# Gate logits with the token blocks as the loaded operand instead of the gate's weights

## Chip, cores and metric

One NeuronCore of a Trainium2 chip runs the whole program. The metric is the device time of one launch in microseconds (us); lower is better.

## What is computed

Three stages in a row, all in fp32 at the interface:

```python
# 1: attention with a memory term: q, k, v of [2, 8, 576, 64]; x becomes [1152, 512]
# 2: a dense layer pair
h = x @ w_in                              # [1152, 2048]
x = softplus(h) @ w_out                   # [1152, 512]
# 3: a mixture of 8 experts, weighted by a balanced matrix
logits = x @ w_gate                       # [1152, 512] @ [512, 8]
P = np.exp(logits - logits.max())
for _ in range(8):
    P /= P.sum(1, keepdims=True) + 1e-09
    P /= P.sum(0, keepdims=True) + 1e-09
    P *= N / E
for e in range(E):
    out += P[:, e:e + 1] * (np.maximum(x @ w1[e], 0.0) @ w2[e])
```

The case is about `logits = x @ w_gate`, the product of 1152 tokens by 8 experts, and about what stands around it in time.

## The kernel before, in words

**Stages.** TensorE works through the attention of 8 pairs of heads, then stage 2 in 2 groups of hidden features by 3 chunks of 384 tokens (N1 = 384), then stage 3. The output of stage 2 is `y1`, laid out with the 512 features on partitions (4 tiles `kt` of 128) and the 1152 tokens along the free axis; it lies in the buffer that is later `acc`, so the trace calls it acc.

**Stage 3.** Every expert is two halves, every half four units u = 0 to 3. The products of x and w1 (`hidden2`) are Strassen-like: seven products "P1" to "P7" of sums of blocks. Units 0 and 1 take tokens 0 to 511 (operands xah, xal, 256 columns wide), units 2 and 3 take tokens 512 to 1151 (operands xbh, xbl, 320 columns wide). Each fp32 product is made of three fp32r products of high and low parts (`products`, line 1525). The result goes to the second product (`output2`, pieces "T0" to "T4", loaded operand zh or zl, 512 columns of w2c moving).

**The order is written out by hand.** TensorE runs, for each unit, the pieces P1, P6, P5, T0, P2, P7, T1, P3, T2, P4, T3, T4, where the P pieces are already those of the next unit and the T pieces those of this one. Each engine has its own list in the same spirit, and they meet at semaphores. Of those that matter here: P2 of a unit waits for `s1_done` (ScalarE has copied P1 out of its bank, `take_s1`), P7 for `u2_done` (VectorE's `sum_u2`, which needs that copy), P6 of the next unit for `h21_done`.

**The gate.** After the last piece of unit 0's hidden product (P3 and P4) TensorE waits for `ld_g` (the gate's weights have landed) and for `y_drained` (VectorE has added the last chunk into y1) and makes the logits expert by token (lines 1757 to 1764): 3 chunks of 384 tokens by 4 feature tiles, 12 matmuls in fp32, the loaded operand being 8 columns of w_gate and the moving one 384 tokens. Chunk 0 goes to the bank `bank_sk` (half of ps_g), chunks 1 and 2 to two banks of ps_y. ScalarE copies the three chunks to `logit_t` in the buffer h_work (`copy_logits`, between the splits `tokens_b` of the operands xbh), each copy signalled in `g_copied`. In the first unit, after piece P5, TensorE waits for all three copies, transposes nine blocks of 8 by 128 back to token by expert in bank_sk (line 1792), and signals `g_tok`. VectorE then takes the maximum (line 1432), further small steps on TensorE (after P7 and P3) and VectorE spread it over the partitions, and ScalarE takes the exponential (line 1043) that the eight balancing rounds start from. `output2` of unit 0 waits for `g_copied` too, since its banks held logits.

**The sums beside it.** While TensorE makes the logits, GpSimd makes four sums of token blocks in order (`token_sums`, lines 663 to 668, tile xbs), ScalarE copies seven operands to xbh (`tokens_b` 0, 1, 2, 3, 4, 6, 5; the last needs the fourth sum) and only then runs `take_s1` of unit 1; VectorE makes the low parts xbl.

```python
            tokens_b(0)
            copy_logits(0)
            tokens_b(1)
            tokens_b(2)
            copy_logits(1)
            tokens_b(3)
            copy_logits(2)
            tokens_b(4)
            tokens_b(6)
            tokens_b(5)
```

Of the kernel before, what the change touches and what calls it, by code (L numbers as in the profile page):

```python
# [13 lines left out]
P = 128  # L14
# [57 lines left out]
def build(nc, q, k, v, M_prev, z_prev, beta, moe_w_in, moe_w_out, moe2_w_gate, moe2_w1, moe2_w2, out):  # L72
    B, H, S, D = q.shape
    DM = H * D
    KT = DM // P
    T = B * S
    E = moe2_w1.shape[0]
# [9 lines left out]
    G1 = moe_w_in.shape[1] // FS  # L87
    C1 = 3
    N1 = T // C1
    NTT = T // P  # L90
# [24 lines left out]
    with ExitStack() as top:  # L115
        def sem(name):
            return top.enter_context(nc.semaphore(name))
# [5 lines left out]
        def at_(name, offset, shape, dt=F32):  # L123

            size = SIZE[dt] * math.prod(shape[1:])
            end = offset + (size + 31) // 32 * 32
            assert end <= LIMIT, (name, end)
            return nc.alloc_sbuf_tensor_at(name, shape, dt, offset=offset), end

        ident, o = at_("ident", BASE, [P, P])  # L130
# [41 lines left out]
        for g in range(G):  # L172
            t_, o = at_(f"pth{g}", o, [P, 2, GKEYS[g], GCOLS[g][1] - GCOLS[g][0]], F32R)
            pth.append(t_)
        for g in range(G):
            t_, o = at_(f"ptl{g}", o, [P, 2, GKEYS[g], GCOLS[g][1] - GCOLS[g][0]], F32R)
# [17 lines left out]
        h_work, o = at_("h_work", X1, [P, 4, N1])  # L194
# [7 lines left out]
        y1 = acc[:, :, :].rearrange("p a b -> p (a b)").rearrange("p (k t) -> p k t", k=KT)  # L202
# [40 lines left out]
        wg, o = at_("wg", o, [P, KT, E])  # L243
# [9 lines left out]
        assert o <= W20 + 5 * DM * 4  # L253
        zh[1], o = at_("zh1", o, [P, 2, 2 * NB], F32R)
        zl[1], o = at_("zl1", o, [P, 2, 2 * NB], F32R)
        logit_t = h_work[0:E, :, :].rearrange("p a b -> p (a b)")

        with ExitStack() as at:
            ps_s = at.enter_context(nc.psum_tensor("ps_s", [P, 4, 512], F32))
# [3 lines left out]
        with ExitStack() as ml:  # L263
            ps_h = ml.enter_context(nc.psum_tensor("ps_h", [P, 2, 512], F32))
            ps_y = ml.enter_context(nc.psum_tensor("ps_y", [P, KT, 512], F32))
            ps_g = ml.enter_context(nc.psum_tensor("ps_g", [P, 2, 512], F32))
        bank_a, bank_b, bank_c = ps_h[:, 0, :], ps_g[:, 0, :], ps_h[:, 1, :]
        bank_sk = ps_g[:, 1, :]
# [16 lines left out]
        def z_bank(u, k):  # L285
            if u < 2:
                return ps_y[:, k, :]
            return bank_sk if k == 0 else ps_y[:, k - 1, :]
# [52 lines left out]

        y_ready = sem("y_ready")
        y_drained = sem("y_drained")
        g_ready = sem("g_ready")
        g_copied = sem("g_copied")
        g_tok = sem("g_tok")
        g_max = sem("g_max")
        g_row = sem("g_row")
# [385 lines left out]
        def _(act):  # L734
# [12 lines left out]
            copy = lambda o, i, **kw: act.activation(o, i, ACT.Copy, **kw)  # L747
# [231 lines left out]
                    act.wait_ge(z_drained, ZT + i + 1)  # L979
                    act.activation(acc[:, i, :], acc[:, i, :], ACT.Copy, scale=weight[:, i, 0:1]).then_inc(scaled, 1)  # L980

            def copy_logits(c):
                act.wait_ge(g_ready, c + 1)
                copy(logit_t[0:E, c * N1:(c + 1) * N1], (bank_sk if c == 0 else ps_y[:, c - 1, :])[0:E, 0:N1])\
                    .then_inc(g_copied, 1)

            def tokens_b(x):
                tokens_hi(x, 2 * NA, NB, xbh, xbs, xb_sum, xb_hi)

# [9 lines left out]
            relu_hi(0, 0, "21")  # L999
            act.wait_ge(y_drained, KT * G1 * C1 + KT)  # L1000
            tokens_b(0)
            copy_logits(0)
            tokens_b(1)
            tokens_b(2)
            copy_logits(1)
            tokens_b(3)
            copy_logits(2)
            tokens_b(4)
            tokens_b(6)
            tokens_b(5)  # L1010
# [469 lines left out]
        def _(pe):  # L1480
# [41 lines left out]
            def products(dst, a, b, start, stop):  # L1522

                for i, (x, y) in enumerate(((0, 0), (0, 1), (1, 0))):
                    last = pe.matmul(dst, a[x], b[y], start=start and i == 0, stop=stop and i == 2)  # L1525
                return last
# [177 lines left out]
            def output2(s, u, k, start):  # L1704

                U, i = 4 * s + u, u % 2
                if k == 0:
                    pe.wait_ge(e_lo, 4 * U + 4)
                    if u < 2:
                        pe.wait_ge(c2_lo, 2 * s + i + 1)  # L1710
                if i == 0:
                    if u == 0:
                        if start:
                            pe.wait_ge(g_copied, min(k + 2, C1))
                        else:
                            pe.wait_ge(z_drained, ZT * s + k - 3)
                    elif k == 0:
                        if start:
                            pe.wait_ge(g_exp, 1)
                        else:  # L1720
                            pe.wait_ge(z_drained, ZT * s - 4)
                    else:
                        pe.wait_ge(z_drained, ZT * s + k)
                cols = slice(k * P, (k + 1) * P)
                for f in range(2):
                    last = products(z_bank(u, k), (zh[u % 2][:, f, cols], zl[u % 2][:, f, cols]),
                                    (w2c_h[i][:, f, :], w2c_l[i][:, f, :]), i == 0 and f == 0, i == 1 and f == 1)
                if k == (TA if u < 2 else TB) - 1:
                    last.then_inc(unit_done, 1)
                elif i == 1:  # L1730
                    last.then_inc(z_ready, 1)
# [23 lines left out]
            hidden2(0, 0, ("P3", "P4"))  # L1755

            pe.wait_ge(ld_g, 16)
            pe.wait_ge(y_drained, KT * G1 * C1 + KT)
            for c in range(C1):
                bank = bank_sk if c == 0 else ps_y[:, c - 1, :]  # L1760
                for kt in range(KT):
                    last = pe.matmul(bank[0:E, 0:N1], wg[:, kt, :], y1[:, kt, c * N1:(c + 1) * N1],  # L1762
                                     start=kt == 0, stop=kt == KT - 1)
                last.then_inc(g_ready, 1)

            def column_sums(it, U):

                if SK_AT[it][1] == "P7":
                    pe.wait_ge(h11_done, U + 2)
                else:  # L1770
                    pe.wait_ge(t12_done, U + 2)
                pe.wait_ge(sk, 8 * it + 4)
                pe.matmul(sums_at(it), ones[:, :], weight[:, :, :].rearrange("p t e -> p (t e)"),
                          start=True, stop=True).then_inc(sk_sum, 1)


            def expert(e, first, last):
                for half in range(2):
                    s, final = 2 * e + half, last and half == 1
                    start = first and half == 0  # L1780
                    for u in range(4):
                        for piece in ("P1", "P6", "P5", "T0", "P2", "P7", "T1", "P3", "T2", "P4", "T3", "T4"):
                            if piece[0] == "T":
                                k = int(piece[1])
                                if k < (TA if u < 2 else TB):
                                    output2(s, u, k, start)
                            elif not (final and u == 3):
                                hidden2(s + (u == 3), (u + 1) % 4, (piece,))
                            if start and u == 0 and piece == "P5":
                                pe.wait_ge(g_copied, C1)  # L1790
                                for i in range(NTT):
                                    t_ = pe.transpose(bank_sk[:, i * E:(i + 1) * E], logit_t[0:E, i * P:(i + 1) * P],
                                                      ident[0:E, 0:E])
                                t_.then_inc(g_tok, 1)
                            if start and u == 0 and piece == "P7":
                                pe.wait_ge(g_max, 1)
                                pe.transpose(bank_sk[0:1, 2 * P:3 * P], sk_max[:, 0:1], ident[:, :]).then_inc(g_row, 1)
                            if start and u == 0 and piece == "P3":
                                pe.wait_ge(g_max, 2)
                                pe.matmul(bank_sk[:, 3 * P:3 * P + 1], ones[0:1, :], sk_max[0:1, 1:2],  # L1800
                                          start=True, stop=True).then_inc(g_all, 1)
                            if first and (4 * s + u, piece) in SK_AT:
                                column_sums(SK_AT.index((4 * s + u, piece)), 4 * s + u)

            expert(0, True, False)
            with pe.Fori(1, E - 1) as e:
                expert(e, False, False)
            expert(E - 1, False, True)


# [21 lines left out]
```

## Time and profile before

| what | value |
|---|---|
| median of 3 runs | 1111.4 us (1110.64 to 1111.64) |
| the profiled execution's own time | 1110.8 us |
| its span, first to last instruction | 1109.0 us |
| TensorE matmuls busy | 1097.5 us (99% of the span), 6698 of them |
| TensorE weight loads busy | 999.2 us (90%) |
| VectorE, ScalarE, GpSimd busy | 704.7, 488.1, 435.2 us |
| mean granted TensorE clock | 1.000 |

PE is TensorE's matmul side and PEld its side that loads the stationary operand; the two overlap. In a row of the trace "ps_y<-acc,wg 128*8 128x384" the output comes first, then the moving operand, then the loaded one; 128*8 is the size of the loaded operand (rows by columns) and 128x384 that of the moving one. An fp32 matmul (as against fp32r) shows as two loads and two matmuls. The ends of matmuls are modelled, so starts of neighbouring rows say more than their durations.

### The profile page before, as it was taken

Reading aid. Unit: us, or ns where it says so; the run is one execution under the profiler, and the core shown is the slowest. Engines: PE = TensorE matmul, PEld = TensorE weight load, DVE = VectorE, ACT = ScalarE, POOL = GpSimd, SP = SyncE. Lnnn points to the kernel's source line nnn. Section 1 sums busy time; section 2 is a strip of 40 time slices with the busy share of each in tenths; the row PEclk is TensorE's granted clock in tenths of the full one; section 3 lists DMA queues with packets and bytes.
Section 4 is the critical chain, followed back from the end, with each engine's and each line's share of the span. In section 5 each row is a group of like instructions: output and inputs, shape, how many; then the busy total and the mean of one; then the engine's idle time right before and its main releaser. Section 6 shows DMA issues by size and latency. Waiting matters only on the chain.

```text
span 1109.0 us, 20425 instructions
## 1 busy us (share of the span) xinstructions
PE 1097.5 (99%) x6698; PEld 999.2 (90%) x6698; DVE 704.7 (64%) x1327; ACT 488.1 (44%) x1069; POOL 435.2 (39%) x486
## 2 busy tenths in 40 slices
PE   7999999999999999999999999999999999999998
PEld 5888999999997989899899898999989898898987
DVE  7999743453278787675756656566665666756564
ACT  6888765664565333433333333333233332333331
POOL 7899700001044334352442524335343442524421
PEclk9999999999999999999999999999999999999999
DMA  5433202001001110111101011110111101111001
GB/s 122 107 96 94 69 29 76 1 27 51 0 20 39 38 58 20 58 58 39 49 27 57 35 41 56 38 57 19 57 57 38 57 19 57 57 38 40 19 10 76
DMA packets 66061, 52.78 MB, mean 48 GB/s; under 512 B 32608, under 2 KB 54112, under 8 KB 66016
## 3 DMA queue, kind: packets, MB, share of 16 engines
q1 hardware_dynamic: 65728, 52.20, 15.3%
q8 instruction: 25, 0.41, 0.2%
q14 instruction: 20, 0.16, 0.0%
q10 hardware_dynamic: 288, 0.01, 0.0%
HBM read 49.83 MB, written 2.36 MB: 47 GB/s over the span
## 4 chain that ended last, share of the span: by engine, by line
PE 95%; DVE 2%; issue 1%; POOL 1%; SPq 1%; DMA 0%; ACT 0%; POOLq 0%; DVEq 0%
PE ps_y L1525 40%; PE ps_h L1525 27%; PE ps_g L1525 17%; PE ps_o L1525 4%; PE ps_p L1567 2%; PE ps_s L1541 2%; PE ps_s L1525 1%; PE ps_y L1762 0%; POOL prob L625 0%; DVE zl L1282 0%; PE ps_t L1505 0%; DVE acc L1402 0%; PE ps_t L1517 0%; PE ps_g L1762 0%; PE ps_t L1510 0%
## 5 line engine op out<-in xcount | busy, mean ns | idle before, releaser
L936 ACT ACTIVATE zh<-h 128x256 fp32r<-128x256 f32 (+1 forms) x256 | 112.2, 444 | 329.4 <-POOL h L698 134.1
L1525 PE MATMUL ps_y<-w2c_h,zh 128*128 128x512 f32 x512 | 202.7, 396 | 0.0
L1525 PE MATMUL ps_y<-w2c_l,zh 128*128 128x512 f32 x512 | 201.8, 394 | 0.0
L1525 PE MATMUL ps_y<-w2c_h,zl 128*128 128x512 f32 x512 | 199.3, 389 | 0.0
L693 POOL TENSOR_TENSOR h<-u,p 128x256 f32<-128x256 f32 (+1 forms) x64 | 56.9, 890 | 362.0 <-DVE u L1259 362.0
L1282 DVE SCALAR_TENSOR_TENSOR zl<-h,zh 128x256 fp32r<-128x256 f32 (+1 forms) x256 | 173.0, 681 | 8.6 <-ACT zh L936 8.5
L1525 PEld LDWEIGHTS ps_y<-w2c_h,zl 128*128 128x128 f32 x512 | 96.2, 188 | 21.9
L1525 PEld LDWEIGHTS ps_y<-w2c_h,zh 128*128 128x128 f32 x512 | 96.6, 189 | 13.5
L1525 PEld LDWEIGHTS ps_y<-w2c_l,zh 128*128 128x128 f32 x512 | 96.6, 189 | 11.8
L1410 DVE SCALAR_TENSOR_TENSOR acc<-ps_y,weight,acc 128x512 f32<-128x512 f32 x112 | 82.0, 741 | 37.2 <-PE ps_y L1525 37.2
L698 POOL TENSOR_TENSOR h<-h,p 128x256 f32<-128x256 f32 (+1 forms) x64 | 60.9, 952 | 101.7 <-DVE h L1270 101.7
L1212 DVE SCALAR_TENSOR_TENSOR h_work<-ps_h,h_work 128x384 f32<-128x384 f32 x48 | 26.7, 557 | 94.4 <-ACT h_work L870 94.4
L1525 PE MATMUL ps_h<-xbh,w1c_l 128*128 128x320 f32 x256 | 79.1, 309 | 0.0
L1525 PE MATMUL ps_h<-xbl,w1c_h 128*128 128x320 f32 x256 | 79.0, 308 | 0.0
L1525 PE MATMUL ps_h<-xbh,w1c_h 128*128 128x320 f32 x256 | 78.6, 307 | 0.0
L686 POOL TENSOR_TENSOR w1c_l<-ws,w1c_h 128x1024 fp32r<-128x1024 f32 x32 | 77.0, 2407 | 0.0
L1525 PE MATMUL ps_h<-xah,w1c_l 128*128 128x256 f32 x256 | 72.4, 283 | 0.0
L1525 PE MATMUL ps_h<-xal,w1c_h 128*128 128x256 f32 x256 | 72.4, 283 | 0.0
L1525 PE MATMUL ps_h<-xah,w1c_h 128*128 128x256 f32 x256 | 72.1, 282 | 0.0
L677 POOL TENSOR_TENSOR ws<-rc 128x256 f32<-128x256 f32 x32 | 25.7, 802 | 117.5 <-DMA rc<-in_moe_w_dram 116.0
L1276 DVE TENSOR_TENSOR h<-ps_g,u 128x256 f32<-128x256 f32 (+1 forms) x64 | 29.3, 458 | 64.5 <-PE ps_g L1525 64.3
L747 ACT ACTIVATE s<-ps_h 128x256 f32<-128x256 f32 (+1 forms) x64 | 26.2, 410 | 96.9 <-PE ps_h L1525 96.8
(248 smaller groups left out, 3031.8 us busy)
## 6 DMA issues: line engine op xcount, KB each, us to landing
rc<-in_moe_w_dram SPq DMA_DIRECT2D x64, 512.0 KB, 3.6
out_dram<-acc SPq DMA_DIRECT2D x9, 256.0 KB, 2.0
q_nat<-in_q_dram SPq DMA_DIRECT2D x16, 128.0 KB, 2.5
k_nat<-in_k_dram SPq DMA_DIRECT2D x16, 128.0 KB, 2.7
v_nat<-in_v_dram SPq DMA_DIRECT2D x16, 128.0 KB, 2.4
raw<-in_moe_w_in_dram SPq DMA_DIRECT2D x8, 256.0 KB, 3.0
raw<-in_moe_w_out_dram SPq DMA_DIRECT2D x8, 256.0 KB, 3.2
raw<-in_moe_w_in_dram SPq DMA_DIRECT2D x1, 2048.0 KB, 8.7
```

The costliest lines, as they stand in the source:

```text
L677: pool.tensor_tensor(ws[:, 0, :, :], a21, a22, ALU.add).then_inc(c1_sum, 1)
L686: pool.tensor_tensor(w1c_l[i][:, 3:7, :, :], ws[:, :, :, :], w1c_h[i][:, 3:7, :, :].bitcast(F32), ALU.subtract).then_inc(c1_los, 1)
L693: pool.tensor_tensor(h22[:, 0:n], u3[:, 0:n], p5[:, 0:n], ALU.add).then_inc(h22_done, 1)
L698: pool.tensor_tensor(h12[:, 0:n], h12[:, 0:n], p5[:, 0:n], ALU.add).then_inc(h12_done, 1)
L747: copy = lambda o, i, **kw: act.activation(o, i, ACT.Copy, **kw)
L936: act.activation(z_place(u, quarter, 0), rows, ACT.Relu).then_inc(e_hi, 1)
L1212: dve.scalar_tensor_tensor(out=h_sp[:, slot % 2, :], in0=ps_h[:, slot % 2, 0:N1], scalar=0.0, in1=h_abs[:, slot % 2, :], op0=ALU.max, op1= ...
L1276: dve.tensor_tensor(h21[:, 0:n], bank_b[:, 0:n], u3[:, 0:n], ALU.add).then_inc(h21_done, 1)
L1282: dve.scalar_tensor_tensor(out=z_place(u, quarter, 1), in0=rows[:, 0:n], scalar=0.0, in1=z_place(u, quarter, 0).bitcast(F32), op0=ALU.max, ...
L1410: dve.scalar_tensor_tensor(out=here, in0=y, scalar=weight[:, i, bass.ds(e, 1)], in1=here, op0=ALU.mult, op1=ALU.add).then_inc(z_drained, 1)
L1525: last = pe.matmul(dst, a[x], b[y], start=start and i == 0, stop=stop and i == 2)
L1541: pe.matmul(ps_s[:, bank + h, 0:w], x[r, half, t * P:(t + 1) * P], y[r, half, 0:w], start=i == 0, stop=False)
```

## The change

The logits are made token by expert at once: for each of the nine blocks of 128 tokens, the block of y1 (128 by 128) is the loaded operand and the 8 columns of w_gate move, 4 feature tiles each, so 36 matmuls. All go to bank_sk, where the transposes used to put their result. The wait for the last chunk of y1 is moved to the first block that reads it (block 6), `g_tok` is signalled by the last matmul, and the copies, the transposes, the buffer view and the two semaphores go.

```diff
-        logit_t = h_work[0:E, :, :].rearrange("p a b -> p (a b)")
...
-            def copy_logits(c):
-                act.wait_ge(g_ready, c + 1)
-                copy(logit_t[0:E, c * N1:(c + 1) * N1], (bank_sk if c == 0 else ps_y[:, c - 1, :])[0:E, 0:N1])\
-                    .then_inc(g_copied, 1)
...
             tokens_b(0)
-            copy_logits(0)
             tokens_b(1)
             tokens_b(2)
-            copy_logits(1)
             tokens_b(3)
-            copy_logits(2)
             tokens_b(4)
...
                     if u == 0:
-                        if start:
-                            pe.wait_ge(g_copied, min(k + 2, C1))
-                        else:
+                        if not start:
                             pe.wait_ge(z_drained, ZT * s + k - 3)
...
             pe.wait_ge(ld_g, 16)
-            pe.wait_ge(y_drained, KT * G1 * C1 + KT)
-            for c in range(C1):
-                bank = bank_sk if c == 0 else ps_y[:, c - 1, :]
+            for i in range(NTT):
+                if i * P == T - N1:
+                    pe.wait_ge(y_drained, KT * G1 * C1 + KT)
                 for kt in range(KT):
-                    last = pe.matmul(bank[0:E, 0:N1], wg[:, kt, :], y1[:, kt, c * N1:(c + 1) * N1],
+                    last = pe.matmul(bank_sk[:, i * E:(i + 1) * E], y1[:, kt, i * P:(i + 1) * P], wg[:, kt, :],
                                      start=kt == 0, stop=kt == KT - 1)
-                last.then_inc(g_ready, 1)
+            last.then_inc(g_tok, 1)
...
-                            if start and u == 0 and piece == "P5":
-                                pe.wait_ge(g_copied, C1)
-                                for i in range(NTT):
-                                    t_ = pe.transpose(bank_sk[:, i * E:(i + 1) * E], logit_t[0:E, i * P:(i + 1) * P],
-                                                      ident[0:E, 0:E])
-                                t_.then_inc(g_tok, 1)
```

## Rows read from the trace of the kernel before

**Rows 1.** The page: TensorE's share, and the chain that ended last by engine.
```profile
PE 1097.5 (99%) x6698; PEld 999.2 (90%) x6698; DVE 704.7 (64%) x1327; ACT 488.1 (44%) x1069; POOL 435.2 (39%) x486
PE 95%; DVE 2%; issue 1%; POOL 1%; SPq 1%; DMA 0%; ACT 0%; POOLq 0%; DVEq 0%
```

**Rows 2.** Groups by line, TensorE: logits (L1762), transposes (L1792); busy us, mean ns.
```profile
L1762 PE MATMUL ps_y<-acc,wg 128*8 128x384 f32 x16 | 5.3, 486 | 0.0
...
L1792 PE MATMUL ps_g<-ident,h_work 8*128 8x8 f32 x9 | 0.7, 204 | 0.0
```

**Rows 3.** Timeline, TensorE, both ends of the logits: start us, us, engine, line.
```profile
342.55 0.28 PE L1525 MATMUL ps_g<-xah,w1c_l 128*128 128x256 f32 x1
342.76 0.10 PEld L1762 LDWEIGHTS ps_g<-acc,wg 128*8 128x8 f32 x2
...
349.86 0.09 PEld L1762 LDWEIGHTS ps_y<-acc,wg 128*8 128x8 f32 x1 [0.23 <-issue]
350.60 0.19 PEld L1525 LDWEIGHTS ps_h<-xah,w1c_h 128*128 128x128 f32 x1 [0.65 <-issue]
```

**Rows 4.** Timeline, TensorE: P5's last matmul, the transposes, T0, P2's first.
```profile
352.62 0.28 PE L1525 MATMUL ps_h<-xal,w1c_h 128*128 128x256 f32 x1
352.74 0.28 PE L1525 MATMUL ps_h<-xah,w1c_l 128*128 128x256 f32 x1
352.95 0.63 PEld L1792 LDWEIGHTS ps_g<-ident,h_work 8*128 8x128 f32 x9
...
353.60 0.19 PEld L1525 LDWEIGHTS ps_y<-w2c_h,zh 128*128 128x128 f32 x1
...
354.86 0.19 PEld L1525 LDWEIGHTS ps_h<-xah,w1c_h 128*128 128x128 f32 x1
355.09 0.28 PE L1525 MATMUL ps_h<-xah,w1c_h 128*128 128x256 f32 x1
```

**Rows 5.** Timeline, TensorE: a small fp32 matmul with a full 128x128 load.
```profile
372.88 0.33 PEld L1773 LDWEIGHTS ps_h<-weight,ones 128*128 128x128 f32 x2
...
373.13 0.19 PEld L1525 LDWEIGHTS ps_y<-w2c_h,zh 128*128 128x128 f32 x1
...
373.24 0.19 PEld L1525 LDWEIGHTS ps_y<-w2c_l,zh 128*128 128x128 f32 x1
```

**Rows 6.** Timeline, ScalarE: a logit copy, the last xbh, take_s1.
```profile
350.71 0.48 ACT L747 ACTIVATE h_work<-ps_y 8x384 f32<-8x384 f32 x1 [1.47 <-PE ps_y L1762]
...
353.39 0.74 ACT L747 ACTIVATE xbh<-xbs 128x640 fp32r<-128x640 f32 x1 [0.95 <-POOL xbs L668]
354.03 0.37 ACT L747 ACTIVATE s<-ps_h 128x256 f32<-128x256 f32 x1
```

**Rows 7.** Timeline, GpSimd's last sum and VectorE's first steps behind it.
```profile
351.21 2.15 POOL L668 TENSOR_TENSOR xbs<-acc 128x640 f32<-128x640 f32 x1
...
354.43 0.42 DVE L1253 TENSOR_TENSOR u<-ps_g,s 128x256 f32<-128x256 f32 x1 [0.39 <-ACT s L747]
...
356.00 0.42 DVE L1264 TENSOR_TENSOR h<-ps_h,s 128x256 f32<-128x256 f32 x1 [0.28 <-PE ps_h L1525]
...
362.50 0.41 DVE L1276 TENSOR_TENSOR h<-ps_g,u 128x256 f32<-128x256 f32 x1
```

**Rows 8.** Windows: us, busy (x) of PE, PEld, DVE, ACT, POOL, PEclk, DMA, GB/s.
```profile
7.00:8.00 1.00, 0.88 (x6) 0.64 (x6) 0.69 (x1) 0.26 (x2) 0.00 (x0) 1.00 0.84 190
8.00:9.00 1.00, 0.00 (x0) 0.00 (x0) 0.60 (x1) 1.00 (x3) 0.00 (x0) 1.00 0.27 58
...
1105.00:1106.00 1.00, 0.73 (x4) 0.27 (x2) 0.39 (x2) 0.00 (x0) 0.00 (x0) 1.00 0.36 139
...
1108.00:1109.00 1.00, 0.00 (x0) 0.00 (x0) 0.00 (x0) 0.00 (x0) 0.00 (x0) 0.55 0.07 25
...
342.60:350.60 8.00, 8.00 (x27) 2.11 (x26) 7.32 (x6) 4.19 (x8) 7.78 (x5) 1.00 0.01 2
```

**Rows 9.** Timeline, TensorE, the first ten matmuls of the program (512 columns each).
```profile
1.54 4.41 PE L1487 MATMUL ps_s<-idle 128*128 128x512 f32 x10 [1.54 <-POOL idle L545]
```

More of the change, by code:

```diff
@@ L343, in build @@
         y_drained = sem("y_drained")
-        g_ready = sem("g_ready")
-        g_copied = sem("g_copied")
         g_tok = sem("g_tok")
```

## The prediction

> **What bounds the kernel now.** I read the page first: TensorE's matmul side is busy 99% of the span and the chain that ended last is 95% TensorE [rows 1]. So time is won only where TensorE's own row of work gets shorter, and lost wherever it waits. The engines beside it count only through waits. Next I read the groups by line, which put a price on what is replaced: the 12 fp32 logit matmuls are 24 records, of which the 16 in ps_y are busy 5.3 us, and 0.7 us for the nine transposes [rows 2]. Then the timeline around both places, because modelled ends overlap and only the starts tell what the path pays. The windows come last, for TensorE's clock.
>
> **Old cost on TensorE's path.** The logits' first load starts at 342.76 and the first load of the next piece at 350.60: 7.84 us [rows 3], or 0.32 us for each of 24 records. That is 384 columns taken twice over at 2.4 GHz, so the streaming of the tokens is the bound and the 8-column loads are idle most of the time ("issue" 0.23 us before each). The entry before it costs little: the last matmul of P4 starts at 342.55, and at the 0.12 us spacing of such 256-column matmuls (352.62 to 352.74 in [rows 4]) the logits could have come at 342.67, so two waits cost 0.09 us. The transposes: P5's last matmul starts at 352.74, where T0's first load would lie if nothing came between (loads start with the matmul ahead of them, 373.13 and 373.24 in [rows 5] being the spacing when nothing hides them). It lies at 353.60 [rows 4]. So transposes and their waits take 0.86 us, of which 0.63 is the nine loads.
>
> **New cost.** 36 fp32 matmuls show as 72 loads of 128 columns and 72 matmuls of 8. The moving side is next to nothing: by the old block's own rate, 0.32 us x 8/384 = 0.007 us. The load becomes the bound. The trace before has no stretch of such pairs, but the nearest rows are close: the column sums of the balancing, fp32, 128x128 loaded, 72 columns moving. Two loads take 0.33 us together at 0.19 each, so the second starts at 373.02; the next load starts at 373.13 and the one after at 373.24 [rows 5]. A full fp32 load follows a small matmul every 0.11 us. 72 x 0.11 = 7.92 us; with the rounding of the rows, 0.106 to 0.112 each, 7.6 to 8.1 us. I take 7.9, against 7.84 before: **the block itself gains nothing**, at best 0.2 and at worst costs 0.3 us. The wait for y_drained moved into it costs what it cost in front of it.
>
> The Trainium skill, in "TensorE: Matmul & The Clock Gate", section "Back-to-back issue gap", gives a measured pace of about 81 ns for load and matmul pairs at 128 columns. By that pace the block would be 72 x 0.081 = 5.8 us, an estimate from the page. The 0.11 us of the fp32 load here disagrees with it, and the measured row decides.
>
> **What the removed parts give.** The transposes go: 0.86 us off TensorE's row. The three copies go from ScalarE, about 0.4 to 0.5 us each [rows 6]; at 350.71 the copy was the last of them, behind an idle 1.47 us. This gives no time by itself, since ScalarE's next deadline is set elsewhere: its last xbh copy waited 0.95 us for GpSimd's fourth sum, which ends at 351.21 + 2.15 = 353.36 [rows 6, 7]. Neither GpSimd's sums nor VectorE's work there wait for logits. g_tok comes 3 us earlier, but VectorE takes the maximum in its list behind sum_u2, which runs at 354.43 when ScalarE's copy is there [rows 7]; nothing follows. No DMA is added, removed or moved.
>
> **What is late next.** P2 of unit 1 needs ScalarE's copy of P1, which starts at 354.03, behind the xbh copy, and ends at 354.40 [rows 6]; with some 0.05 us of signalling, P2's load can start at about 354.45. Before, that load started at 354.86 [rows 4], so there was 0.4 us of slack. With 0.86 us gone and the block 0.08 longer, TensorE would come to it at 354.08 and now waits about 0.4 us; its load, hidden before, then stands open, and the matmul follows at 354.45 + 0.11 = 354.56 instead of 355.09 [rows 4]. **So 0.5 us is what arrives, and it is a cap**: the GpSimd chain does not move with TensorE, however fast the logits get. It also means that a block up to 0.4 us longer than I take costs nothing. Behind it VectorE was waiting for TensorE (0.28 us at 356.00), so it moves up by about that; result_21 at 362.50 + 0.41 [rows 7] would end near 362.65, in time for P6 of unit 2, which came at 363.6 less 0.5. From there on VectorE has waits for TensorE again and the lead is kept to the end.
>
> **The sum.** Block +0.08, transposes -0.86, new wait for ScalarE +0.25 net: -0.53 us. Against the profiled execution's 1110.8 us (span 1109.0 and 1.8 around it) that is 1110.3. That execution lies 0.6 us under the median of the runs, 1111.4; so the median to expect is **1110.9 us**. About 0.2%, 2.2 us, is what a measurement of this kernel can tell from no change, so this is "the same". Its own range is 1110.2 to 1111.7: the bounds of the block, plus the scatter of the runs shown (1.0 us).
>
> **Rivals.**
>
> *A: the clock falls (slower).* In the new block TensorE loads all the time but streams about 0.007 us in 0.11, for 8 us on end. The rows before have no such stretch: the logits ran at a granted clock of 1.00 with the matmul side streaming throughout [rows 8]. They do show that idleness brings the clock to its 1.2 GHz level: the last matmuls end at about 1105.7, and 1108 to 1109 has a mean of 0.55 [rows 8], so the clock fell at about 1108.1, 2.4 us after. And they show what recovery takes: the first ten matmuls take 4.41 us, (4.41 - 0.62 for the last)/9 = 0.42 us each for 512 columns, which is the 1.2 GHz level (1.54 us in, [rows 9]), so some 4 us of dense work come before full speed. Price: if it falls 2.4 us into the block, the remaining 5.5 us cost as much again, and 4 us of dense work afterwards cost 2 more; if it falls at the block's very end, only those 2. With the 0.86 us gained: +1.2 to +6.7, middle +4, so 1115.4 us (1112.6 to 1118.1). It decides on whether loading counts as work for the clock. For: by streaming alone the block is nearly idle. Against: loads and matmuls are under way in every moment of it; and in 7 to 9 us the clock stayed at 1.00 with few 128-column transposes and then a whole idle microsecond [rows 8]. Two bounds and no row between them: 0.43.
>
> The Trainium skill, same page, "Part 4: PE-mode transpose", says that transposes do not count as busy for the clock as matmuls do. The 1.00 over 7 to 9 us does not bear that out, since only transposes stood there; but by such a rule a stretch of loads with hardly any stream would count for little too, and give rival A's time.
>
> *B: the load is quicker than I take (faster).* The nine loads of the transposes take 0.63 us, 0.07 each [rows 4]. At that pace the block is 72 x 0.07 = 5.0 us and TensorE is 0.86 + 2.8 = 3.7 us early. But then P2 waits for the same copy at 354.40, and the gain is still 0.5 us. To get over 2.2 us, GpSimd's chain would have to speed up by 1.7 as well, for which nothing speaks. 0.03.
>
> *C: load and matmul do not overlap.* Then each pair costs up to 0.11 + 0.1 us for the matmul to get through, the block is 15 us and the time 1118. Against: in [rows 4] nine pairs with 8 moving columns run at 0.07 us although each matmul lasts 204 ns [rows 2], so they do overlap. 0.02.
>
> *D: the change doesn't do what it says.* That the block still shows 24 records, or copies remain; the diff leaves no room. Under 0.01.
>
> **How the numbers follow.** Forecast (same) 0.52, A 0.43, C 0.02, B 0.03. A's lowest part (a fall late in the block) would count as same, but the forecast has a tail above as well; I leave same at 0.53, slower 0.44, faster 0.03. The predicted time is the forecast's. The range needs both cases: from 1110.2 to 1116.8 it leaves out the lowest twentieth of the forecast, the top fifth of A and C.
>
> **What the profile after would show.** 72 loads and 72 matmuls on the new line, from about 342.7 to 350.6, starts 0.11 us apart; no L747 copies of h_work; T0's load straight after P5; a wait of P2 for ScalarE of 0.3 to 0.5 us near 354; the span near 1108.5. If A is right: granted clock under 1.00 in the window from 342.6 to 360, loads 0.2 us apart from some point on, 256-column matmuls 0.24 us apart after. I am wrong if the block is not load-bound, or if the stall at P2 is absent while the 0.86 us show up whole.

## The result: slower by half a per cent, and the profile after

| | before | changed |
|---|---|---|
| median, 6 runs each | 1111.2 us (1110.64 to 1111.64) | 1116.29 us (1115.13 to 1117.04) |
| ratio | | 1.0045, 95% interval 1.0032 to 1.0058 |
| span of the profiled execution | 1109.0 us | 1115.2 us |
| mean granted TensorE clock | 1.000 | 0.993 |

5.1 us were lost where 0.5 were forecast to be won. The profiled execution of the changed kernel is the slowest of its six (1117.04 us), so its span is 6.2 us longer than the one before, not 5.1. The page of the changed kernel, TensorE's part and the granted clock in 40 slices:

```profile
PE 1102.9 (99%) x6737; PEld 1010.8 (91%) x6737; DVE 704.3 (63%) x1327; ACT 487.0 (44%) x1066; POOL 435.1 (39%) x486
PEclk9999999999997999999999999999999999999999
PE 95%; DVE 2%; issue 1%; SPq 1%; POOL 1%; DMA 1%; ACT 0%; POOLq 0%; DVEq 0%
```

By shares and chain next to nothing has changed against [rows 1]: TensorE is still busy 99% of the span and still is 95% of the chain. The one line that differs is the granted clock, in its thirteenth slice. The windows around it, changed kernel (us, then busy of PE, PEld, DVE, ACT, POOL, then PEclk, DMA share, GB/s):

```profile
342.60:345.00 2.40, 2.40 (x24) 2.40 (x23) 1.56 (x5) 0.74 (x3) 1.61 (x2) 1.00 0.05 15
345.00:347.00 2.00, 2.00 (x16) 2.00 (x16) 2.00 (x2) 1.86 (x3) 2.00 (x2) 0.77 0.00 0
347.00:349.00 2.00, 2.00 (x11) 2.00 (x11) 2.00 (x2) 0.74 (x1) 1.92 (x2) 0.50 0.00 0
...
355.00:357.00 2.00, 2.00 (x11) 2.00 (x11) 0.00 (x0) 0.00 (x0) 0.00 (x0) 0.50 0.00 0
357.00:360.00 3.00, 3.00 (x17) 3.00 (x17) 0.81 (x3) 0.38 (x1) 0.00 (x0) 0.54 0.00 0
360.00:365.00 5.00, 5.00 (x33) 4.40 (x31) 2.93 (x7) 2.17 (x4) 0.79 (x1) 1.00 0.00 0
```

From the means the clock drops to its 1.2 GHz level at 346.1 (0.77 over 345 to 347) and is back at 2.4 GHz at 359.8 (0.54 over 357 to 360): 13.7 us at the low level. The counts of instructions say it too: 24 matmuls and 23 loads in the first 2.4 us, 11 of each in 2 us once the clock is low. Busy shares say nothing, all of them are full. TensorE's timeline of the same stretch:

```profile
343.29 0.28 PE L1514 MATMUL ps_g<-xah,w1c_l 128*128 128x256 f32 x1
343.29 12.94 PEld L1749 LDWEIGHTS ps_g<-wg,acc 128*128 128x128 f32 x72
...
356.11 0.33 PEld L1514 LDWEIGHTS ps_h<-xah,w1c_h 128*128 128x128 f32 x1
...
358.46 0.42 PE L1514 MATMUL ps_g<-xal,w1c_h 128*128 128x256 f32 x1
358.67 0.42 PE L1514 MATMUL ps_g<-xah,w1c_l 128*128 128x256 f32 x1
...
359.86 0.19 PEld L1514 LDWEIGHTS ps_y<-w2c_h,zh 128*128 128x128 f32 x1
...
361.13 0.19 PEld L1514 LDWEIGHTS ps_h<-xah,w1c_h 128*128 128x128 f32 x1
361.36 0.28 PE L1514 MATMUL ps_h<-xah,w1c_h 128*128 128x256 f32 x1
368.97 0.31 PE L1514 MATMUL ps_h<-xbh,w1c_h 128*128 128x320 f32 x1
```

The 72 loads take 12.8 us, from 343.29 to the next load at 356.11; in [rows 3] the block took 7.84. A narrower window of the weight loads shows the first part at full clock, 25 loads in 2.91 us or (2.91 - 0.19)/24 = 0.113 us each:

```profile
343.29 2.91 PEld L1749 LDWEIGHTS ps_g<-wg,acc 128*128 128x128 f32 x25
```

The other 47 take (356.11 - 343.29 - 25 x 0.113)/47 = 0.213 us each, 1.9 times as long. The 256-column matmuls behind are 0.21 us apart (358.46, 358.67) instead of 0.12, 1.8 times as long. So the loads slow down with the clock nearly as much as the matmuls do, and neither takes quite twice as long. Once the clock is back, T0 to P2 run as they should, and nothing idles ahead of P2 (its load at 361.13): TensorE is by then so late that ScalarE's copy has long been made.

For an account that leaves the scatter of the attention stage out (0.7 us in these two profiles, 342.55 against 343.29), I take one stretch in all kernels below: from the last matmul of P4 (before: 342.55 in [rows 3]; changed: 343.29) to the first 320-column matmul, unit 2's P1. Before it is at

```profile
362.73 0.30 PE L1525 MATMUL ps_h<-xbh,w1c_h 128*128 128x320 f32 x1
```

so the stretch is 20.18 us before and 368.97 - 343.29 = 25.68 us changed, 5.50 more. The rest of the program is as long as before (1109.0 - 362.73 = 746.3 and 1115.2 - 368.97 = 746.2).

### The profile page after: what moved, and what is told of

Same layout as the page of the kernel before. It is cut to its first block, busy times and chain, and to the rows that moved or that the text cites. A ratio compares the mean times of both kernels' runs of the same rounds, so it can differ in the third digit from the quotient of the medians.

```text
span 1115.2 us, 20499 instructions
## 1 busy us (share of the span) xinstructions
PE 1102.9 (99%) x6737; PEld 1010.8 (91%) x6737; DVE 704.3 (63%) x1327; ACT 487.0 (44%) x1066; POOL 435.1 (39%) x486
## 4 chain that ended last, share of the span: by engine, by line
PE 95%; DVE 2%; issue 1%; SPq 1%; POOL 1%; DMA 1%; ACT 0%; POOLq 0%; DVEq 0%
PE ps_y L1514 40%; PE ps_h L1514 27%; PE ps_g L1514 17%; PE ps_o L1514 4%; PE ps_p L1556 2%; PE ps_s L1530 2%; PE ps_g L1749 1%; DMA mem_nat<-in_M_prev_dram 1%; PE ps_s L1514 0%; DVE zl L1271 0%; PE ps_t L1494 0%; DVE acc L1391 0%; PE ps_t L1506 0%; PE ps_t L1499 0%; SPq L449 0%
```

## The experiments

Theory 1: the clock falls because next to nothing streams through TensorE while it loads. Theory 2: it is the kind or number of instructions (8 us of full fp32 loads), however many columns they stream. The forecast's own steps, a block of 7.9 us and a gain capped by a wait for ScalarE, wanted a test as well.

### Streaming more without doing more

The loaded operands, instructions and waits stay as in the change; the moving operand is repeated R times, its copies written side by side in the same bank and never read.

```diff
-                    last = pe.matmul(bank_sk[:, i * E:(i + 1) * E], y1[:, kt, i * P:(i + 1) * P], wg[:, kt, :],
+                    last = pe.matmul(bank_sk[:, 0:R * NTT * E].rearrange("p (r c) -> p r c", r=R)[:, :, i * E:(i + 1) * E],
+                                     y1[:, kt, i * P:(i + 1) * P], wg[:, kt, :].unsqueeze(1).to_broadcast([P, R, E]),
                                      start=kt == 0, stop=kt == KT - 1)
```

R = 7, 56 columns, expected:

> The changed kernel, but each logit matmul moves the gate's 8 columns seven times over (56 columns, seven copies side by side in the same bank; only the first is read). Loads, instructions, order and waits are those of the changed kernel. Theory 1 (the clock falls because almost nothing streams): streaming 56 columns takes 0.05 us (0.32 x 56/384) and stays hidden behind the 0.11 us load, the clock stays at 1.00, the block takes 7.9 us as forecast, first load of the block to first load of T0 is 10.0 us (before 10.84, changed 16.57), median 1110.4 to 1111.0. Theory 2 (the clock falls because of 8 us of back-to-back full fp32 loads, or of so many short instructions, whatever they stream): the clock falls as in the changed kernel, first load to T0 16 to 17 us, median about 1116.3. If theory 1 holds it also shows whether P2 of unit 1 waits for ScalarE's copy at all: forecast a matmul start 0.2 to 0.3 us later than the 0.23 us spacing of T0's matmuls would give.

Measured: 1110.85 us, before beside it 1110.78, ratio 0.9998 (0.9988 to 1.0008). One of its ten runs took 3178.32 us at a mean clock of 1.00; nothing on record says why, and the ratio leaves it out. Windows of its profile, 344 to 352 us, of which the two in the middle read 1.00 as well, and the timelines of TensorE and ScalarE:

```profile
344.00:346.00 2.00, 2.00 (x21) 2.00 (x19) 1.57 (x1) 2.00 (x5) 2.00 (x1) 1.00 0.00 0
...
350.00:352.00 2.00, 2.00 (x20) 2.00 (x20) 2.00 (x2) 0.65 (x2) 2.00 (x2) 1.00 0.00 0
```
```profile
343.00 0.28 PE L1514 MATMUL ps_g<-xah,w1c_l 128*128 128x256 f32 x1
343.12 8.14 PE L1749 MATMUL ps_g<-wg,acc 128*128 128x56 f32 x72
...
354.47 0.39 PE L1514 MATMUL ps_y<-w2c_h,zl 128*128 128x512 f32 x1
355.00 0.35 PE L1514 MATMUL ps_h<-xah,w1c_h 128*128 128x256 f32 x1
...
362.69 0.30 PE L1514 MATMUL ps_h<-xbh,w1c_h 128*128 128x320 f32 x1
```
```profile
343.00 8.13 PEld L1749 LDWEIGHTS ps_g<-wg,acc 128*128 128x128 f32 x72
351.05 0.19 PEld L1514 LDWEIGHTS ps_h<-xah,w1c_h 128*128 128x128 f32 x1
...
353.19 0.19 PEld L1514 LDWEIGHTS ps_y<-w2c_h,zh 128*128 128x128 f32 x1
...
354.24 0.19 PEld L1514 LDWEIGHTS ps_y<-w2c_h,zl 128*128 128x128 f32 x1
354.97 0.19 PEld L1514 LDWEIGHTS ps_h<-xah,w1c_h 128*128 128x128 f32 x1 [0.54 <-issue]
```
```profile
353.85 0.74 ACT L744 ACTIVATE xbh<-xbs 128x640 fp32r<-128x640 f32 x1 [1.38 <-POOL xbs L665]
354.49 0.37 ACT L744 ACTIVATE s<-ps_h 128x256 f32<-128x256 f32 x1
```

The same 72 loads and the same number of matmuls, more columns, and the clock stays at 1.00 over the block: theory 2 is out. It is not one execution's luck: the mean clock of the whole run was 0.998 to 1.000 in all ten runs here, and 0.992 to 0.995 in the six of the changed kernel. The block takes 8.05 us (343.00 to 351.05), 0.112 per load, and the stretch 362.69 - 343.00 = 19.69 us, 0.49 less than before; the forecast was 0.53. The median does not show it: a gain of this size is within the interval. The idle 0.54 us ahead of P2's load is the wait that was forecast, at about 0.4: ScalarE's copy s runs from 354.49 to 354.86, behind the xbh copy that waited for GpSimd, and the load follows at 354.97.

R = 3, 24 columns, expected:

> The same with three copies (24 columns moving, 0.02 us of streaming per 0.11 us load). Theory 1 expects something between the changed kernel (8 columns, fell) and the one with 56: most likely the clock still falls and the time is 1115 to 1117. Theory 2: falls as in the changed kernel, 1116.3. If it does not fall, 1110.4 to 1111.0, little streaming is enough.

Measured: a single run, 1115.47 us (before 1110.78). The clock falls, 5.6 us after the first load (343.36 to 348.9) instead of 2.8. With one profile of each, it is not shown that the columns make it later:

```profile
346.00:348.00 2.00, 2.00 (x21) 2.00 (x20) 2.00 (x2) 0.93 (x2) 2.00 (x2) 1.00 0.00 0
348.00:350.00 2.00, 2.00 (x16) 2.00 (x15) 2.00 (x2) 0.74 (x1) 1.90 (x2) 0.73 0.00 0
350.00:352.00 2.00, 2.00 (x11) 2.00 (x11) 2.00 (x2) 0.74 (x1) 1.95 (x1) 0.50 0.00 0
```

R = 5, 40 columns, together with the step of ScalarE's list that is told below, expected:

> As the 56-column version with ScalarE's step moved, but five copies of the gate's columns (40 moving). If the clock stays at 1.00 it is the same as with 56 columns, since the load of 0.11 us is the bound in both: first logit load to first 320-column matmul 19.3 us, median 0.3 to 0.85 under before. If the clock falls: 1114 to 1117, as with 24 columns. From the 56- and 24-column runs both can be; I give 6 in 10 to the fall staying away.

Measured: 1115.14 us (1112.96 to 1115.32), ratio 1.0036 (1.0023 to 1.005). It falls too, so my 6 in 10 were on the wrong side. The profiled execution is the quickest of its runs, with the clock low for 6.8 us:

```profile
348.00:350.00 2.00, 2.00 (x13) 2.00 (x12) 2.00 (x2) 0.84 (x2) 1.92 (x2) 0.56 0.00 0
...
354.00:356.00 2.00, 2.00 (x14) 2.00 (x14) 0.57 (x3) 0.38 (x1) 0.00 (x0) 0.74 0.00 0
```

(0.56 puts the fall at 348.2, 0.74 the return at 355.0.) So without ScalarE's step 8 and 24 columns lost the clock and 56 kept it; with that step 40 lost it and 56 kept it (in the next version, all eleven runs with a mean clock of 0.998 to 1.000, against 0.993 to 0.997 in the five with 40).

### ScalarE's step

The seventh xbh copy is moved behind the two copies of unit 1 that TensorE waits for.

```diff
             tokens_b(6)
-            tokens_b(5)
...
                         take_s1(V, v)
                         if new:
                             weights_hi(s + 1, u % 2, 1)
                         take_p5(V, v)
+                        if start and u == 0:
+                            tokens_b(5)
```

With 56 columns, expected:

> The 56-column version with one step of ScalarE's list moved: the seventh xbh copy (tokens_b(5), the one that waits for GpSimd's fourth sum) comes behind take_s1 and take_p5 of unit 1 instead of ahead of them. Theory (the gain is capped at 0.5 us because P2 waits for a ScalarE copy queued behind GpSimd's chain): P2's load now starts with T0's last matmul and no idle time stands before it (0.54 us in the 56-column version), so 0.3 us more arrive: first load of the block to the first 320-column matmul is 19.3 to 19.5 us (before 19.97, 56 columns 19.69), median 0.3 us under that of the 56-column version, 0.5 to 0.8 under before. Rival (what P2 waits for is VectorE or the matmuls' own semaphores): the idle time stays.

Measured: 1110.48 us (1109.84 to 1110.75), before beside it 1110.81, ratio 0.9993 (0.9984 to 1.0002): not told apart from before by the interval. The profile shows the step itself:

```profile
342.47 0.28 PE L1515 MATMUL ps_g<-xah,w1c_l 128*128 128x256 f32 x1
...
353.94 0.39 PE L1515 MATMUL ps_y<-w2c_h,zl 128*128 128x512 f32 x1
354.17 0.28 PE L1515 MATMUL ps_h<-xah,w1c_h 128*128 128x256 f32 x1
...
361.78 0.30 PE L1515 MATMUL ps_h<-xbh,w1c_h 128*128 128x320 f32 x1
```

P2's first matmul follows T0's last after 0.23 us (0.53 with the wait), and the stretch is 361.78 - 342.47 = 19.31 us, 0.38 less again and 0.87 less than before. The wait was behind ScalarE's list; the rival is out. In the totals it shows blurred: the runs of each kernel seem to lie in two groups some 0.6 us apart, before 1110.67 to 1110.81 and from 1111.07 up, this one 1109.84 to 1109.97 and 1110.48 to 1110.75. Group against group it is about 0.8 us, but these groups were formed after the fact, and that reading proves nothing by itself.

The same step in the kernel before, expected:

> The kernel before with only ScalarE's seventh xbh copy moved behind take_s1 and take_p5 of unit 1, the logits, copies and transposes as before. Theory (the move matters only once the transposes are gone, since P2's load at 354.86 was 0.4 us behind what it waited for): no change within 0.1 us, first logit load to the first 320-column matmul 19.97 us as before. Rival (the move gains by itself, so that the 56-column version with the move owes 0.4 us of its gain to it alone): 0.3 to 0.5 us under before.

Measured: 1110.85 us, before beside it 1110.88, ratio 0.9999 (0.9990 to 1.0008). Its first 320-column matmul comes 363.06 - 343.09 = 19.97 us after the first logit load, as before (362.73 - 342.76). As expected: before, the wait was covered.

```profile
343.09 2.75 PE L1763 MATMUL ps_g<-acc,wg 128*8 128x384 f32 x8
...
363.06 0.30 PE L1526 MATMUL ps_h<-xbh,w1c_h 128*128 128x320 f32 x1
```

### The same matmuls in other places

8 columns again. `gate_block(i)` holds the change's loop body for one block of tokens.

```diff
+                    if g == G1 - 1 and last_chunk and s in EARLY:   # EARLY = {2: [0], 3: [1], ..., 7: [5]}
+                        pe.wait_ge(ld_g, 16)
+                        pe.wait_ge(y_drained, KT * (C1 + 2) + KT)
+                        for i in EARLY[s]:
+                            gate_block(i)
...
+                            if start and u == 0 and piece in LATE:  # LATE = {"P1": [6], "P6": [7], "P5": [8]}
+                                for i in LATE[piece]:
+                                    gate_block(i)
```

Expected:

> The changed kernel's matmuls as they are (8 columns moving), but the nine token blocks are not in one row: blocks 0 to 5 go one by one between the steps 2 to 7 of the last chunk of stage 2, blocks 6, 7 and 8 behind the pieces P1, P6 and P5 of the first unit. Each is 8 loads or 0.9 us. Theory 1: the clock stays at 1.00 since dense matmuls stand around every block; total on TensorE's path as forecast, median 1110.4 to 1111.2. Theory 2 (loads or short instructions of themselves): 72 loads are still there but never 8 us in a row, so it expects the same if only a row counts; it expects a fall if the sum counts, near 1113 to 1116.

Measured: 1117.65 us, ratio 1.0061 (1.0044 to 1.0077), against the expectation and slower than the change. Its windows, TensorE's waits over 340 to 365 us (us in total, times, longest), and the first step of GpSimd's chain here and in the kernel before:

```profile
330.00:335.00 5.00, 5.00 (x34) 5.00 (x33) 1.71 (x3) 2.59 (x5) 0.00 (x0) 1.00 0.00 0
...
348.00:350.00 2.00, 2.00 (x19) 1.95 (x17) 1.31 (x4) 0.77 (x3) 1.65 (x2) 1.00 0.00 0
350.00:352.00 2.00, 0.48 (x4) 0.44 (x4) 2.00 (x2) 1.83 (x3) 2.00 (x2) 1.00 0.00 0
352.00:354.00 2.00, 2.00 (x17) 2.00 (x16) 2.00 (x2) 0.74 (x1) 1.92 (x2) 0.82 0.00 0
```
```profile
PE ps_g L1514 <- POOL w1c_l L683: 1.5, 1, 1.5
PE ps_h L1514 <- ACT s L744: 1.2, 1, 1.2
```
```profile
349.16 2.35 POOL L683 TENSOR_TENSOR w1c_l<-ws,w1c_h 128x1024 fp32r<-128x1024 f32 x1
```
```profile
343.46 2.34 POOL L686 TENSOR_TENSOR w1c_l<-ws,w1c_h 128x1024 fp32r<-128x1024 f32 x1
```

Through all the blocks that stand among stage 2's matmuls the clock is 1.00, as theory 1 has it. What no theory had foreseen: TensorE idles 1.5 us for GpSimd at 350 to 351.6, the clock falls behind that at about 353.3, and P2 waits 1.2 us for ScalarE. GpSimd's chain (low part of w1c, then the four sums) starts behind `result_12` of unit 0, which needs unit 0's hidden product, so about when TensorE has got through that product: at 343.46 before, with the first logit load at 342.76, and at 349.16 here, with block 6's first load at 348.97. The logits used to stand behind that moment and gave the chain 8 us; six of the nine blocks have now been done ahead of it. The block was cover. This run therefore does not settle what clumping alone does.

Blocks 0 to 5 in one row ahead of step 3 of stage 2's last chunk, 6 to 8 in one row at the old place, expected:

> The same matmuls in two rows: blocks 0 to 5 together (48 loads, 5.3 us) ahead of step 3 of the last chunk of stage 2, blocks 6 to 8 together (24 loads, 2.6 us) where the whole block was. Theory 1: a row of 5.3 us is probably still enough to lower the clock, near its end; then the loads behind the fall and about 4 us of dense work take twice as long, 1113 to 1115. If neither row lowers it, 1110.4 to 1111.2, and the length of the row is what decides. The row of 2.6 us alone should not lower it.

Measured: a single run, 1120.36 us, outside every time expected. The row of 48 loads (from 320.77) does lower the clock, at 325.5 and so near its end as expected, and TensorE, again without cover, then idles 5.0 us for ScalarE at P2:

```profile
325.00:330.00 5.00, 5.00 (x23) 5.00 (x23) 0.00 (x0) 0.00 (x0) 0.00 (x0) 0.55 0.00 0
...
352.00:354.00 2.00, 2.00 (x19) 2.00 (x20) 1.55 (x1) 2.00 (x5) 2.00 (x1) 1.00 0.00 0
354.00:356.00 2.00, 2.00 (x18) 1.93 (x17) 2.00 (x2) 0.61 (x1) 2.00 (x2) 1.00 0.00 0
```
```profile
PE ps_h L1514 <- ACT s L744: 5.0, 1, 5.0
```

The row of 24 loads (350 to 353) left it at 1.00; a second fall, at about 363, comes behind the 5.0 us of waiting.

To keep the cover, all nine blocks behind unit 0's product with unit 1's and 0's pieces between them (blocks 0, 1, P1, 2, 3, P6, 4, 5, P5, 6, T0, 7, 8), expected:

> 8 columns moving as in the changed kernel, all 72 loads behind the same point, but with the first unit's dense pieces between them: blocks 0 and 1, P1, 2 and 3, P6, 4 and 5, P5, 6, T0, 7 and 8, then P2 as before. So the same work stands in front of P2 and GpSimd's chain keeps its cover, which the spread version took away. Theory 1 (a long stretch in which hardly anything streams is what lowers the clock): stays at 1.00, nothing idle before P2 beyond what the 56-column version shows, median 1110.3 to 1111.0. Rival (the total of such loads, or the kind of load, lowers it): falls, 1115 or more.

Measured: 1117.3 us (1113.7 to 1119.42), ratio 1.0055 (1.0035 to 1.0075), against the expectation. TensorE waits for nobody here, yet:

```profile
346.00:348.00 2.00, 2.00 (x19) 2.00 (x20) 2.00 (x3) 0.58 (x2) 1.92 (x2) 1.00 0.00 0
348.00:350.00 2.00, 2.00 (x14) 2.00 (x13) 2.00 (x2) 1.00 (x2) 1.92 (x2) 0.60 0.00 0
...
360.00:362.00 2.00, 2.00 (x12) 1.91 (x11) 0.74 (x2) 0.71 (x2) 0.00 (x0) 0.50 0.00 0
```

The clock falls at 348.4, although nowhere ahead of it more than two blocks (16 loads, 1.85 us) stand together. So theory 1 as I had put it, a long unbroken row, is too narrow: dense pieces of 0.7 us between blocks of 1.8 us did not hold the clock either. It was low for 13.7 us in this execution (348.4 to 362.1), as long as in the change, with blocks 7 and 8 in that time. Beside the 40-column run, this fits a cause in how little streams over the stretch as a whole, and not in rows; that is an argument, and no run shows it by itself.

## Why the prediction was wrong

**Old cost, new cost, what goes.** Right while the clock is up, as the 56-column version shows. 0.11 us a load was forecast, 0.112 measured; a block of 7.9 us, 8.05 measured; nothing won in the block itself, which costs 0.21 us more than before, not 0.08. One small term was missing: the new block's first load starts together with P4's last matmul (both at 343.00), where the old one came 0.21 us behind it [rows 3]. So the two cancel, and the transposes' 0.86 us are the gain: 0.87 measured.

**What is late next, the cap.** Right, by the 56-column version: -0.49 us in the stretch for the forecast -0.53, with the idle time in front of P2, at ScalarE's copy; with ScalarE's step moved the stretch wins 0.87. The wait so takes back 0.38 us, for 0.25 in the sum.

**The step that failed** is the choice between forecast and rival A. The sum took each load at 0.11 us for all 72, a price from rows with dense matmuls on both sides [rows 5], and I gave 0.52 to a clock that stays and 0.43 to one that falls, for want of a row between the two. That price failed: the block took 12.82 us, and P1, P6 and P5 behind it 3.75 (356.11 to 359.86) instead of 2.14 (351.05 to 353.19 with 56 columns). The mechanism of A happened, by the signs named for it: loads 0.21 us apart (0.2 named), 256-column matmuls 0.21 apart behind them (0.24 named). I had counted the presence of loads in every moment as a ground against it. The runs say that it is none: the clock fell 2.8 us after the first load of the block (343.3 to 346.1), about as soon as after the last matmul of the program, 2.4 us [rows 8], when TensorE did nothing. The quiet stretch at 7 to 9 us was no ground either: in the profiles of the 56-column version and of the kernel before with ScalarE's step, whose programs begin alike, the granted clock was 0.50 from 10 to 12 us, right behind it. That the trace at hand did not show this was luck. Nor is a granted clock of 1.00 so early in a trace safe by itself: it also stands over the first ten matmuls, which were 0.42 us apart.

**A's price** was 1115.4 us in the middle, 1112.6 to 1118.1; measured 1116.29. The fall came 2.8 us into the block, near the early end that was priced (2.4), and the return 3.7 us after the block's end (356.1 to 359.8), where 4 was taken. A took time at the low level to cost twice as much. It costs 1.9 times as much for the loads and 1.8 for the matmuls, and with that the sum closes: 12.82 - 8.05 = 4.77 us lost in the block and 3.75 - 2.14 = 1.61 behind it, less the 0.87 that the change gains when P2 has nothing to wait for, make 5.51 us; the stretch shows 5.50.

**The range**, 1110.2 to 1116.8, holds the median; the direction was wrong, and the chances leaned the wrong way: 0.53 on the same, 0.44 on slower.

The rule of the Trainium skill that I had set beside rival A ("TensorE: Matmul & The Clock Gate", "Part 4: PE-mode transpose": transposes do not count as busy for the clock) was not tested by any run here. The Trainium skill, same page, "Part 1: The HAM clock gate", says that the clock is given by how busy the engine has been; by that rule these runs agree only if loading with hardly anything to stream is not taken for busy. The pace of about 81 ns that the Trainium skill gives there in "Back-to-back issue gap" for a pair at 128 columns was not seen: fp32 loads came every 0.112 us.

## What to carry to other kernels

Swapping the operands of a thin matmul swaps its bound: 24 records of 0.32 us streaming and 72 records of 0.11 us loading took about the same time here (7.84 and 8.05 us at full clock), and only the second left TensorE with almost nothing to stream. Before doing so, ask what the clock will do, and price it with the dense work behind; if the load is the bound, try to widen the moving side under it: 56 columns cost no time in the block here and kept the clock, and with ScalarE's step 0.87 us were won in the stretch, though the medians do not tell that gain from none. And before work is moved forward past a point in the program, look which other engine's chain starts at that point: a block on the busiest engine may be the time that another engine's chain needs.

## What the runs showed of the hardware

- At the 1.2 GHz level a full fp32 load took 0.213 us instead of 0.113, so loading depends on the clock nearly as streaming does (changed kernel, 47 and 25 loads; the 256-column matmuls 0.21 instead of 0.12).
- Back-to-back loads with 8 columns moving did not keep the clock up: it fell 2.8 us after they began, with PEld busy all the time, and stayed low for 13.7 us. The same loads with 56 columns moving ran at 1.00.
- For how long the clock is low differs between executions of one program: the interleaved version took 1113.7 to 1119.42 us at mean clocks of 0.996 to 0.991, the one with 40 columns 1112.96 to 1115.32 at 0.997 to 0.993. Not every kernel in which it falls scatters so widely: the spread version took 1117.01 to 1117.91.
